# Block transposes of r on VectorE instead of TensorE, with new slots for the decays and two slots for v

## What is computed

```
for t in range(S):
    cur = einsum('bhd,bhe->bhde', u[None] * kt, vt)
    y[:, :, t] = einsum('bhd,bhde->bhe', rt, state + cur)
    state = wt[:, :, :, None] * state + einsum('bhd,bhe->bhde', kt, vt)
```

## Time and profile before

| | us |
|---|---|
| median of 3 runs (836.99 to 837.52) | 837.47 |
| the profiled execution | 837.12 |
| its span from first to last instruction | 835.2 |
| busy: TensorE, VectorE, ScalarE, GpSimd | 814.3, 571.3, 439.1, 205.5 |
| a group of the steady stretch (scores at 302.59 and 369.53) | 66.9 |

### The profile page before, as it was taken

The page is one execution under the profiler, slowest core; times in us unless marked ns, Lnnn a source line. Parts: engine busy times, 40 slices in busy tenths (PEclk is TensorE's granted clock), DMA queues, the critical chain, the costliest instruction groups (busy, mean ns, idle before and its releaser), DMA issues.

```text
span 835.2 us, 18049 instructions
## 1 busy us (share of the span) xinstructions
PE 814.3 (97%) x5633; PEld 764.3 (92%) x5633; DVE 571.3 (68%) x1315; ACT 439.1 (53%) x924; POOL 205.5 (25%) x286
## 2 busy tenths in 40 slices
PE   6999999999999999999999999999999999999997
PEld 5899999999989999999999999999989999898896
DVE  6889699789889788979878865636361512545563
ACT  5676464364464465455446435654563533555563
POOL 5611111121103012112112001212353322424433
PEclk9999999999999999999999999999999999999999
DMA  9976233145233123223221000513531512475392
GB/s 205 201 163 144 35 68 58 34 85 85 42 68 44 26 37 66 51 37 67 55 35 39 1 16 30 171 38 112 191 124 39 186 47 80 153 257 188 104 306 75
DMA packets 165306, 78.55 MB, mean 94 GB/s; under 512 B 135486, under 2 KB 153253, under 8 KB 165090
## 3 DMA queue, kind: packets, MB, share of 16 engines
q1 hardware_dynamic: 156402, 64.81, 31.8%
q0 software_dynamic: 4544, 10.85, 4.0%
q10 hardware_dynamic: 4272, 1.82, 1.0%
HBM read 112.90 MB, written 11.63 MB: 149 GB/s over the span
## 4 chain that ended last, share of the span: by engine, by line
PE 80%; DVE 8%; issue 4%; ACT 3%; DMA 1%; ACTq 0%; SPq 0%; DVEq 0%; POOL 0%; POOLq 0%
PE bank L1058 20%; PE bank L1037 19%; PE bank L1110 13%; PE bank L1146 13%; PE bank L963 3%; PE bank L1127 3%; PE bank L991 2%; PE bank L986 2%; PE bank L930 2%; DVE Fi L1639 1%; PE bank L971 1%; DVE Xi L1655 1%; PE bank L1092 1%; DVE gl L1726 1%; PE bank L1000 1%
## 5 line engine op out<-in xcount | busy, mean ns | idle before, releaser
L1037 PE MATMUL bank<-xhl,WRh 128*128 128x384 f32 x768 | 218.9, 339 | 0.2 <-issue 0.2
L1037 PEld LDWEIGHTS bank<-xhl,WRh 128*128 128x128 f32 x768 | 141.2, 188 | 0.4 <-issue 0.4
L1058 PE MATMUL bank<-WRh,gh 128*128 128x384 f32 x384 | 135.8, 354 | 0.0
L1404 ACT COPY gw<-bank 128x384 f32<-128x384 f32 x128 | 61.5, 480 | 132.3 <-PE bank L1037 132.2
L1037 PE MATMUL bank<-xhl,WRl 128*128 128x384 f32 x384 | 130.0, 339 | 0.0
L1058 PE MATMUL bank<-WRh,gl 128*128 128x384 f32 x384 | 129.8, 338 | 0.0
L1058 PE MATMUL bank<-WRl,gh 128*128 128x384 f32 x384 | 129.7, 338 | 0.0
L1410 ACT CAST gh<-gw 128x384 fp32r<-128x384 f32 x128 | 65.5, 512 | 97.3 <-DVE gw L1719 82.9
L1719 DVE SCALAR_TENSOR_TENSOR gw<-gw 128x384 f32<-128x384 f32 x128 | 72.6, 567 | 50.5 <-ACT gw L1404 50.3
L1726 DVE TENSOR_TENSOR gl<-gw,gh 128x384 fp32r<-128x384 f32 x128 | 79.0, 617 | 34.0 <-ACT gh L1410 29.5
L1894 DVE TENSOR_TENSOR hl<-bank,hh 128x512 fp32r<-128x512 f32 x56 | 36.1, 686 | 84.6 <-ACT hh L1445 84.2
(11 more groups left out here) (199 smaller groups left out, 1644.7 us busy)
## 6 DMA issues: line engine op xcount, KB each, us to landing
stage<-in_moe_w_dram SPq DMA_DIRECT2D x96, 768.0 KB
Kn<-in_k_dram SPq DMA_DIRECT2D x24, 192.0 KB, 3.5
Vn<-in_v_dram SPq DMA_DIRECT2D x24, 192.0 KB, 3.6
x_moe<-x2s SPq DMA_DIRECT2D x24, 192.0 KB, 3.0
Rn<-in_r_dram SPq DMA_DIRECT2D x21, 192.0 KB, 2.8
wraw<-in_moe_w_out_dram SPq DMA_DIRECT2D x4, 768.0 KB, 7.5
eraw<-in_moe_w_dram SPq DMA_DIRECT2D x4, 768.0 KB, 9.0
Wn<-in_w_dram SPq DMA_DIRECT2D x152, 16.0 KB, 1.8
```

Of the source, the lines that this page charges most:

```text
L1037: mm = pe.matmul(bank[F_BANK[n % 2]][:, 0:GN], win(t_)[:, f // 4, k_, cols], xhl[G % 2][:, a, k_, :], start=(k_ == 0 and n_ == 0), stop=(k ...
L1058: mm = pe.matmul(bank[O_BANK[i]][:, 0:DM], a[:, z, cols], wout(t_)[:, f, :], start=(f == 0 and n_ == 0), stop=(f == FT - 1 and n_ == 2))
L1404: act.copy(gw[:, n % 2, :], bank[F_BANK[n % 2]][:, 0:GN]).then_inc(s_g0, 1)
```

## The change

- r of chunks 5 to 23 is loaded a second time, in blocks, into two new slots of `Rn` (`next_r`, 16 DMAs), and turned by VectorE into `Rh` itself (`turn_r`), directly before the multiply, which then reads and writes `Rh`. The four transposes of r on TensorE go for these chunks. The plain load of r stays, for GpSimd's products, in two slots instead of three.
- GpSimd clears the two new slots once (`s_pad`).
- v has two slots instead of three; its loads are issued later by one chunk.
- On VectorE the block transpose of w, the forward scan and the backward scan have slots of their own (`BLOCK_SLOTS`, by chunk of the group), instead of following `turn_w_at`. ScalarE's check of w and SP's loads in blocks follow them.

```
-        Vn = sb("Vn", [P, NSLOT, H, HEAD_PAD], c=att)
+        Vn = sb("Vn", [P, 2, H, HEAD_PAD], c=att)
...
+        BLOCK_SLOTS = ((-5, -3, -2), (0, 2, 4), (6, 8, 9))
...
+            block_at[m_], decay_to_at[m_], decay_from_at[m_] = [FT * (g_ - 1) + x for x in BLOCK_SLOTS[i_]]
...
                 sp.wait_ge(s_kT, m - NSLOT + 1)
-                sp.wait_ge(s_rk, m - NSLOT + 1)
+                sp.wait_ge(s_rk, m - NSLOT + 1 if m < BLOCKED else m - 1)
...
+            def next_r(m):
+
+                if m == BLOCKED:
+                    sp.wait_ge(s_pad, 1)
+                if m > BLOCKED + 1:
+                    sp.wait_ge(s_rT, m - 1)
+                load_blocks(sp, m, r, Rn, r_blocks(m), s_rblk[m % 2])
...
             load_weights(0)
             next_load(GT)
-            next_v(GT)
+            next_v(GT - 1)
             load_weights(1)
...
             next_load(GT + 1)
+            next_v(GT)
             load_weights(2)
             next_v(GT + 1)
             load_weights(3)
             next_load(GT + 2)
-            next_v(GT + 2)
             next_w(GT + 2)
+            next_r(GT + 2)
...
                 for m in at(sum_at, n - 1):
                     if m % GT == GT - 1:
                         fill(m // GT)
-                    if m + NSLOT < NC:
-                        next_v(m + NSLOT)
-                    if m % GT == GT - 1 and m + 2 < NC:
+                    if m + 2 < NC:
+                        next_v(m + 2)
+                if n == turn_w_at[GT + 1] + 4:
+                    next_w(GT + 3)
+                for m in blocks(block_at, n - 3):
+                    if m + 2 < NC:
                         next_w(m + 2)
+                for m in at(turn_at, n - 2):
+                    if GT < m and m + 2 < NC:
+                        next_r(m + 2)
                 for m in at(turn_w_at, n - 4):
-                    if GT < m and m % GT < GT - 1 and m + 2 < NC:
-                        next_w(m + 2)
                     if m + NSLOT < NC:
                         next_load(m + NSLOT)
...
+            pool.wait_ge(s_rT, NSLOT)
+            pool.memset(Rn[:, NSLOT - 1:NSLOT + 1].rearrange("p s h d -> p (s h d)"), 0.0).then_inc(s_pad, 1)
...
-                turn_one(m, Rn, banks(m)[1], s_rT)
+                if m < BLOCKED:
+                    turn_one(m, Rn, banks(m)[1], s_rT)
...
-                return turn_w_at.get(m, -3) + 3
+                return block_at[m] + 1 if m >= BLOCKED else turn_w_at.get(m, -3) + 3
...
+            def turn_r(m):
+
+                dve.wait_ge(s_rblk[m % 2], 16 * 4 * HP * ((m - BLOCKED) // 2 + 1))
+                dve.wait_ge(s_ym, m - 1)
+                dve.transpose(Rh[:, m % 2].rearrange("p h t -> p (h t)"),
+                              Rn[:, r_blocks(m)].rearrange("p h d -> p (h d)")).then_inc(s_rT, 1)
...
-                dve.tensor_tensor(Rh[:, m % 2], pair(b_), Fi[:, m % 2, :, 0:P], ALU.mult).then_inc(s_rh, 1)
+                dve.tensor_tensor(Rh[:, m % 2], Rh[:, m % 2] if m >= BLOCKED else pair(b_), Fi[:, m % 2, :, 0:P], ALU.mult).then_inc(s_rh, 1)
...
+                        for m in blocks(decay_to_at, n):
+                            decay_to(m)
+                        for m in blocks(decay_from_at, n):
+                            decay_from(m)
...
-                            if m >= BLOCKED:
-                                turn_w(m)
                             bonus_sum(m)
+                        for m in blocks(block_at, n):
+                            turn_w(m)
```

More of the change, by code:

```diff
@@ L193, in build @@
         s_nat = [sem(f"s_nat{i}") for i in range(NSLOT)]
-        s_vin = [sem(f"s_vin{i}") for i in range(NSLOT)]
+        s_vin = [sem(f"s_vin{i}") for i in range(2)]
+        s_rblk = [sem(f"s_rblk{i}") for i in range(2)]
+        s_pad = sem("s_pad")
         s_wT = sem("s_wT")
@@ L243, in w_slot, with r_slot, r_blocks @@
             return m % NSLOT if m < BLOCKED else (m - BLOCKED) % 2
+        def r_slot(m):
+            return w_slot(m)
+        def r_blocks(m):
+            return 2 + (m - BLOCKED) % 2
         def w_loaded(m):
@@ L264, in build, with blocks @@
                 FT * (g_ - 1) + x for x in (FIRST_SLOTS if g_ == 1 else SLOTS)[i_]]
+            block_at[m_], decay_to_at[m_], decay_from_at[m_] = [FT * (g_ - 1) + x for x in BLOCK_SLOTS[i_]]
         def at(table, n):
             return [m for m in range(GT, NC) if table[m] == n]
+        def blocks(table, n):
+            return [m for m in range(BLOCKED, NC) if table[m] == n]
         moves = x2s[:, 2, 0:KT * HEAD_PAD].rearrange("p (k c) -> p k c", k=KT)
@@ L1494, in mlp @@
                             split_hi(2 * (n // 4) + n % 4)
-                        for m in at(turn_w_at, n - 3):
-                            check_decays(m)
+                        for m in range(GT, NC):
+                            if check_slot(m) == n:
+                                check_decays(m)
                     if not first and n == FT + 3:
@@ L1661, in decay_rk @@
                 a_, b_, c_ = banks(m)
+                if m >= BLOCKED:
+                    turn_r(m)
                 dve.wait_ge(s_rT, m + 1)
@@ L1961, in mlp @@
                         light = not any(at(t_, n - 1) for t_ in (turn_at, score_at, sum_at))
-                        some = 0 if at(turn_w_at, n - 1) or (f == 3 and G > 1) else 3 if light else 2
+                        some = 0 if f in (4, 9, 14) or (f == 3 and G > 1) else 3 if light and f != 8 else 2
                         if f == FT - 1:
```

43 lines of the change are left out of this document (23 added, 20 removed).

## The result

Medians of four runs each, taken in turn on one chip: 849.34 us for the changed kernel (848.25 to 850.3), 837.5 for the kernel before. The ratio is 1.0142, with a 95% interval of 1.0126 to 1.0157: slower by about 11.8 us. The forecast was 842.3, slower by 4.8: the sign holds, and so do nearly all the places, but the size is less than half of what came. The profiled execution took 848.25 us, 11.15 more than that of the kernel before.

A forecast was written before the change was run, and what follows sets the result against it. TensorE was taken to bound the kernel, busy 814.3 of 835.2 us. Profiled execution 837.1 + 12.8 (SP's queue) - 7.6 (transposes) - 4.0 (first chunks) + 4.0 (second chunks) = 842.3 us; range 828 to 856.

The forecast's parts named there:

- SP's queue in the first group: SP's in-order issue before the second group's fill: added blocks land it at 108.8 instead of 96.06, 12.8 us lost.
- I took 7.8 us per chunk, nearer the quiet rows: SP's first-group queue: assumed issue time of each set of sixteen block DMAs, because the weights are through by then.
- half of w5 gets through: SP's queue from 45.46: half of w5 issues in V's former 5.43 us, the rest at normal rate, ending at 56.
- Rival 4: TensorE after its two waits: slower matmuls again, adding up to 3 us, some hidden in the second wait; no chance given.
- the first wait lies within the second and not on top: TensorE, first group: sums start 7.7 us late behind w6's transpose, within the 12.8; then about 5 us more for the fill.
- Removed from TensorE: Four transposes of r gone in chunks 5 to 23, 0.42 us each, chunk 5 not counted: 7.6 us gained.
- the first chunks: First chunk of a group: VectorE's new slots remove the scores' wait in chunks 9, 12, 15, 18, 21, 4.0 us gained.
- The second chunks: Second chunk of a group: Kt late from the transpose and held Rh; 0.8 us each in five chunks, 4.0 us lost.
- the waits of L963: Sign of being right: the scores' waits sit at second chunks, near 0.8 us, and are gone at first ones.
- Rivals 1 and 2: SP's lateness misses TensorE, 823.6 or 827.6 us (chance 0.14); or half of it, fill at 102 to 104, 835 to 838 (0.16).
- Rival 3: SP short in the next five groups too, fill or transpose 2 to 4 us late each: 852 to 862 us, chance 0.12.
- The estimate of 855 us: First group: at the skill's descriptor-bound pace, 64 extra DMAs need 44 us instead of 31, loss 26; shares rival 3's chance.

The follow-up runs named there:

- e5: Changed kernel plus idle transposes on TensorE in its two stands of the first group (76 before the mask wait, 46 before the fill wait): 848.37 us.
- e12: Changed kernel with r in blocks from chunk 7 on instead of 5, one chunk of r blocks ahead of the first fill: 832.28 us.
- e3: Changed kernel with the same transfers in another order on SP's queue, w6 ahead of r6 and r7 behind the fill: 844.48 us.
- e1: Changed kernel with its VectorE slots and v in two slots, but r as before the change, turned by TensorE in every chunk: 833.29 us.
- e7: Changed kernel with y's low part, from chunk 5 on, ahead of the feature's low part and the state's sum on VectorE: 849.02 us.
- e9: From e8, GpSimd's two products for the third chunk of a group wait for Kt of the second: 826.1 us.
- e10: From e8, VectorE's block transpose of r at second chunks moved ahead of gl, into VectorE's idle time: 825.95 us.
- e6: Changed kernel with the blocks of r for chunks 5, 6 and 7 issued by GpSimd on its own queue instead of SP: 842.3 us.
- e2: Changed kernel with r in blocks and turned by VectorE from chunk 9 on instead of chunk 5: 829.8 us.
- e8: Changed kernel with r in blocks from chunk 8 on and y's low part first on VectorE: 828.73 us.

## Why the forecast was right in direction and wrong in size

**SP's queue in the first group: right mechanism, 12.8 us charged, 19.4 measured.** This is the step that failed, in two terms.

| | forecast | measured |
|---|---|---|
| w5 issued | 56 | 57.6 |
| r5 issued | 63.6 | 65.4 |
| embb, loads, V through | 70.8 | 72.7 |
| r6 issued | 78.6 | 81.6 |
| w6 issued | 86.4 | 89.2 |
| fill issued from | 105 | 109.2 |
| first feature of the second group | 108.8 | 113.0 |

The first term is the pace: "I took 7.8 us per chunk, nearer the quiet rows". The five sets of blocks behind w5 took 41.1 us, 8.2 each; they make 2.1 of the 4.2 us by which the fill is late against the forecast. w5 makes another 1.6: "half of w5 gets through" in the time of the V that stood there, so the forecast gave it 10.5 us, to 56 (its own terms, 5.43 and half of 8.7, come to 9.8 and 55.2). It took 12.7, and between 12.4 and 13.95 in all twelve experiments, beginning at 44 to 46 us each time. The earlier trace rows had V at 5.43 and w5 at 8.68, 14.1 together, and that sum was the safer reading: in every kernel the first transfers issued at this place were slow. The forecast says that the rings were full there; no run shows the rings. What the traces show is that the DMA engines were busy throughout from 30 to 50 us, when the large loads of weights ran, and that w5 stayed slow to 57.6. What holds SP there, and why w5 varies by 1.5 us between runs, stays open.

The second term is the clock. Rival 4 named it ("up to 3 us, some of it hidden in the second wait") and the sum left it out. It added 2.4 us to slot 16; e5 took it away and e12 showed it behind a stand of 1.93 us. The part behind the first stand is hidden by the wait for the fill, as forecast. A stand that is in the sum should bring its slow stretch into the sum.

The order of events was right: VectorE's stand at w6 (79.0 to 88.2 forecast, 80.3 to 90.7 measured), the sums from 92.8 (94.8), then 4 to 5 us more for the fill (6.2). That the first wait lies within the second and not on top holds: e3 cut it by 6.7 us, and slot 16 moved by 5.3, as the fill's issue did (5.4).

**Removed from TensorE, 7.6, and the first chunks, 4.0: right.** At the first chunks 4.0 us of waits are gone in e1 and in the changed kernel. The 7.6 has not been measured by itself, only the sum it stands in. e1 has the slots alone at 4.1 us between slots 17 and 127. From there to the changed kernel, which gives up the r transposes for the block transposes, it is 446.1 less 441.5, 4.6 us more; the forecast had 7.6 - 4.0 = 3.6.

**The second chunks, 4.0: near in size by luck, wrong in the wait that costs it.** The forecast put 0.8 us at the scores of five chunks. The trace has 4.8 us at k's transposes in six and none at the scores. It is another wait, with another cause, that happens to cost about as much. The step that was missed is who covered what: the removed transposes of r stood ahead of those of k and covered the wait for y's low part. e7 took that wait away and met the forecast one, 3.2 us in the five chunks. Its two parts are the ones named, GpSimd holding `Rh` and the transpose in front: e9 took away the first, e10 both but at chunk 16. One detail was wrong: gl is not held, it ends before the products begin. Of two waits in a row the second shows only as far as the first leaves it. The prediction named the waits of L963 as its sign, and that sign is missing in the changed kernel though `Rh` is held there.

The Trainium skill's rule on the products (GPSIMD Engine Reference, section 8, Key points), that GpSimd contends with VectorE instructions with two SBUF inputs, agrees with every row here: `Rh` from PSUM 0.68 in the earlier trace rows, from SBUF 1.11 to 2.06 beside the products, 0.69 without them.

**Rivals 1 and 2** fall: the fill landed at 113. **Rival 3** was not far off: the 158 us that SP waited between 100 and 460 us have shrunk to

```profile
SPq L591 <- DVE xhl L1734: 14.1, 4, 4.8
SPq L544 <- PE bank L1036: 9.2, 4, 3.3
```

and yet no fill of a later group is late in this execution; in e3 two were (1.14 and 0.38 us), in e5 one (0.97) and in e6 one (0.28). The estimate of 855 us, which took the Trainium skill's 0.68 us for 4 KB (DMA: Bandwidth & Descriptors, section Bandwidth) as the pace, doesn't hold: behind w5 a set of sixteen was out in 7.5 to 9 us.

**The account.** Of the 7.0 us between forecast and measurement 4.2 are the fill's lateness, 2.4 the slow slot 16. 0.6 came behind the last slot, and 1.1 is the distance of the runs' median from the profiled execution, for which the sum was made. Against them stand the 1.2 that the second part gained beyond the forecast's 7.6. Together 7.1.

## What to carry to other kernels

A queue that issues in order has to be summed up to each transfer that someone waits for, with the rates of the crowded rows, and the last transfer wanted (here three small ones of 48 KB) should not stand behind prefetches that are due later: the same change begun three or four chunks later turned a loss of 12 us into a gain of 7.3 (e2) and 8.6 (e8). When an edit takes work off the bound engine, look for what that work covered; and when a wait goes without the time moving, look where the next one is before you call the edit useless. Work given to a second engine goes where it idles, not in front of the instruction that the bound engine waits for: that, or keeping GpSimd away from one product, brought another 2.6 to 2.8 us.

## What the runs showed of the chip

- A stand of 1.93 us on TensorE was followed by some 3.5 us at the lower clock level (e12, listed 0.52 a matmul instead of 0.34; granted clock 0.85 in 95 to 100 us and 0.81 in 100 to 105). The stands of 1.14 us in e3 at 176 us and in e5 at 114 us were not: those slots lasted 3.3 us.
- GpSimd takes 0.55 us of its own time to issue one transfer of 8 or 16 KB (17.64 us for 32, 8.71 for 16) and computes nothing meanwhile; SP takes 0.47 to 0.58 (7.46 to 9.23 us for 16), apart from the set below.
- A set of sixteen on SP took 12.4 to 13.95 us right behind the large loads of weights (thirteen kernels), 7.46 in a quiet stretch.
- VectorE's product with two SBUF inputs was stretched from 0.69 to up to 2.06 us (e10, chunk 16) with GpSimd's two products beside it, and took 0.69 in all 16 chunks of e9, where they were kept away. With one input in PSUM it kept 0.68 beside them.
